# Attention followed by two feed-forward layers on one core: probabilities turned two tiles behind their scores, with four ring buffers

## What is computed

```python
scores = scale * q @ k.T + bias            # bias: relu(x @ w1 + b1) @ w2
attn = exp(scores - max); attn = attn / (sum(attn) + 1e-9)
o = attn @ v                               # 32 (batch, head) pairs of 576 x 64
h = max(x @ w1, x @ w2, x @ w3)            # x: 2304 x 512, h: 2304 x 768
x2 = h @ w_out
h2 = x2 @ w_in                             # 2304 x 2048
g = where(h2 >= 1, h2, where(h2 <= -1, 0, (h2 + 1)**2 / 4))
out = g @ w_out2
```

## Time and profile before

| | us |
|---|---|
| median of three runs | 1044.38 (1044.34 to 1044.47) |
| the profiled execution | 1044.05 |
| its span in the trace | 1042.0 |
| TensorE busy in the span | 1004.5 |
| VectorE, ScalarE, GpSimd busy | 504.7, 496.9, 293.3 |

### The profile page before, as it was taken

One profiled execution on the slowest core, in us unless ns is written; L12 is line 12 of the kernel. 1 busy time (PEld: TensorE's weight loads), 2 busy tenths in 40 slices (PEclk: granted clock), 3 DMA queues, 4 the chain that ended last, 5 costly groups with the idle time before them and its releaser, 6 DMA issues.

```text
span 1042.0 us, 20386 instructions
## 1 busy us (share of the span) xinstructions
PE 1004.5 (96%) x7608; PEld 865.7 (83%) x7608; DVE 504.7 (48%) x1172; ACT 496.9 (48%) x1024; POOL 293.3 (28%) x510
## 2 busy tenths in 40 slices
PE   6759999999998999999999999999999999999998
PEld 4447666666665999999999999998989989899997
DVE  8846666766765232313232315754454444544443
ACT  8867777877776321212121325543343443433433
POOL 1037888888874630000000234800000000000000
PEclk9978999999999999999999999999999999999999
DMA  5872432534411320000000022300000000000000
GB/s 140 260 205 65 131 83 57 151 69 127 121 25 42 122 81 1 1 0 0 0 0 0 24 73 66 122 1 31 1 31 0 0 30 0 30 0 0 31 1 31
DMA packets 96042, 56.10 MB, mean 54 GB/s; under 512 B 64224, under 2 KB 81632, under 8 KB 95968
## 3 DMA queue, kind: packets, MB, share of 16 engines
q1 hardware_dynamic: 95872, 55.11, 18.8%
q10 hardware_dynamic: 96, 0.00, 0.0%
HBM read 39.46 MB, written 15.63 MB: 53 GB/s over the span
## 4 chain that ended last, share of the span: by engine, by line
PE 89%; DMA 3%; issue 2%; ACT 2%; DVE 1%; SPq 1%; POOL 1%; ACTq 0%; DVEq 0%
PE ps L1032 41%; PE ps L1092 19%; PE ps L984 7%; PE ps L1060 7%; PE ps L932 7%; PE ps L945 4%; DMA bias_scratch<-p_t 3%; PE ps L959 1%; PE ps L908 1%; DVE s_sb L757 1%; ACT p_t L554 1%; ACT xT L545 1%; POOL probs L495 1%; PE ps L1018 1%; DMA k_in<-in_k 0%
## 5 line engine op out<-in xcount | busy, mean ns | idle before, releaser
L1032 PE MATMUL ps<-x_hi,w_all 128*128 128x384 f32 x1632 | 437.1, 336 | 1.5 <-issue 1.5
L1032 PEld LDWEIGHTS ps<-x_hi,w_all 128*128 128x128 f32 x1632 | 296.9, 188 | 6.7 <-issue 2.5
L1032 PE MATMUL ps<-x_lo,w_all 128*128 128x384 f32 x816 | 273.2, 335 | 0.0
L1092 PE MATMUL ps<-w_all,g_hi 128*128 128x512 f32 x576 | 179.7, 393 | 0.0
L514 POOL TENSOR_TENSOR w_all<-raw,w_all 128x256 fp32r<-128x256 f32 x104 | 80.2, 804 | 271.9 <-ACT w_all L637 267.2
L1032 PEld LDWEIGHTS ps<-x_lo,w_all 128*128 128x128 f32 x816 | 153.2, 188 | 3.9
L757 DVE CUSTOM_DVE_ANT_0 s_sb<-ps,bias_h 128x576 f32<-128x576 f32 (+1 forms) x160 | 114.6, 753 | 59.5 <-PE ps L932 51.2
L578 ACT ACTIVATE probs<-s_sb,row_min 128x576 f32<-128x576 f32 (+1 forms) x160 | 123.0, 769 | 5.2 <-DVE row_min L757 5.2
L1092 PEld LDWEIGHTS ps<-w_all,g_hi 128*128 128x128 f32 x576 | 106.3, 188 | 19.3 <-issue 1.2
L495 POOL TENSOR_SCALAR probs<-probs,row_inv 128x576 f32<-128x576 f32 (+1 forms) x160 | 117.8, 747 | 8.1 <-DVE row_inv L787 8.1
L1092 PE MATMUL ps<-w_all,g_lo 128*128 128x512 f32 x288 | 113.9, 396 | 0.0
(11 more groups left out here) (78 smaller groups left out, 1338.1 us busy)
## 6 DMA issues: line engine op xcount, KB each, us to landing
bias_scratch<-p_t SPq DMA_DIRECT2D x36, 296.0 KB, 3.9
raw<-in_moe_w_out SPq DMA_DIRECT2D x22, 256.0 KB, 3.1
bias_h<-bias_scratch SPq DMA_DIRECT2D x16, 288.0 KB, 4.0
raw<-in_moe_w SPq DMA_DIRECT2D x18, 256.0 KB, 3.1
out<-o_sb SPq DMA_DIRECT2D x18, 256.0 KB, 2.1
q_in<-in_q SPq DMA_DIRECT2D x32, 128.0 KB, 2.4
bias_h<-bias_scratch SPq DMA_DIRECT2D x16, 256.0 KB, 3.3
v_in<-in_v SPq DMA_DIRECT2D x32, 128.0 KB, 2.4
```

The lines of the kernel that those rows point to most:

```text
L1032: last = pe.matmul(ps[:, bank, 0:BLK], w[:, at:at + P], x[:, kt, :], start=(kt == 0 and n == 0), stop=(kt == KT - 1 and n == 2))
L1092: last = pe.matmul(ps[:, O_BANK + t, :], g[:, ft % 4, t * P:(t + 1) * P], w[:, wout_d(ft):wout_d(ft) + DM], start=(opens and i == 0), stop ...
```

## The change

LAG goes from 3 to 2 and the ring from 5 to 4. Within a slot, TensorE now runs `turn_probs` ahead of `turn_rest`, and ScalarE runs `copy_upper`, `copy_turned` and then both exponents. The `VALUES` table spreads 8, 12, 8, 8 and 4 matmuls over a group's slots, in place of 8, 8, 4, 12 and 8. q and k of group 2 are loaded ahead of the last bias loads and of v. The first block of x and the first two weight units are split in slots 71 to 79, and the first two `first_item` stand in slots 80 and 81. GpSimd's slot keeps its order.

```diff
--- before.py
+++ after.py
@@ -44,7 +44,7 @@
     PAIRS = B * H
     GROUPS = PAIRS // 2
     NU = GROUPS * NT
-    LAG = 3
+    LAG = 2
     RING = LAG + 2
     KT = DM // P
     BLK = 384
@@ -196,6 +196,7 @@
 
         SLOTS = range(NU + LAG)
         TURN = 10
+        X_SPLIT, W_SPLIT = NU - 9, NU - 5
         HALVES = (slice(0, HALF), slice(HALF, P))
 
         def ring(s):
@@ -378,6 +379,7 @@
                 if s > 4 and (s - 4) % 8 == 0:
                     first_bias(1, (s - 4) // 8 - 1, s - 4)
             first_bias(1, T - 1, NSUP - 4)
+            load_qk(2)
             for h in range(2):
                 first_bias(h, T, NSUP)
             sp.wait_ge(staged_zero, 1)
@@ -409,7 +411,7 @@
                 sp.dma_start(dst, b).then_inc(raw_in[e], 16)
 
             for i in range(GROUPS):
-                if i + 2 < GROUPS:
+                if 1 <= i < GROUPS - 2:
                     load_qk(i + 2)
                 if i:
                     load_v(i)
@@ -518,9 +520,6 @@
             for w in range(NU + 1):
                 slot(w)
 
-            pool.wait_ge(w_ok, 1)
-            low_weights(1)
-            pool.wait_ge(o_ok, PAIRS)
             pool.wait_ge(w_ok, 3)
             for u in range(3, U1 + U2):
                 low_weights(u)
@@ -612,12 +611,11 @@
                 last.then_inc(t_cp, 1)
 
             def slot(w):
+                if tile_of(w) is not None:
+                    copy_upper(tile_of(w))
                 copy_turned(w)
                 if w < NU:
                     exponent(w, 0)
-                if tile_of(w) is not None:
-                    copy_upper(tile_of(w))
-                if w < NU:
                     exponent(w, 1)
 
             def split_x(b, used, product, per_block, hi_ok):
@@ -627,7 +625,11 @@
                         act.wait_ge(used, (KT - 1) * (b - 1) + kt + 1)
                     elif used is not None:
                         act.wait_ge(product, per_block * b)
-                    act.activation(x_hi[:, kt, :], xT[:, kt, ds(b * BLK, BLK)], ACT.Copy).then_inc(hi_ok, 1)
+                    high_x(b, kt, hi_ok)
+
+            def high_x(b, kt, hi_ok):
+
+                act.activation(x_hi[:, kt, :], xT[:, kt, ds(b * BLK, BLK)], ACT.Copy).then_inc(hi_ok, 1)
 
             def split_weights(u):
                 at = unit_at(u)
@@ -645,11 +647,12 @@
                 bias_copy(s)
             for w in SLOTS:
                 slot(w)
-                if w == NU - 1:
-                    split_x(0, None, None, 0, c_x_hi)
-                if w == NU:
-                    split_weights(0)
-            split_weights(1)
+                if w == X_SPLIT:
+                    act.wait_ge(o_ok, 2 * (GROUPS - B) + 2)
+                if X_SPLIT <= w < X_SPLIT + KT:
+                    high_x(0, w - X_SPLIT, c_x_hi)
+                if w in (W_SPLIT, W_SPLIT + 2):
+                    split_weights((w - W_SPLIT) // 2)
             act.wait_ge(o_ok, PAIRS)
 
             split_weights(2)
@@ -788,7 +791,7 @@
 
             def slot(w):
                 i, t = w // NT, w % NT
-                if t == 3 and i >= 1:
+                if t == 2 and i >= 1:
                     output(i - 1, 0)
                 if t == 0 and i >= 2:
                     output(i - 2, 1)
@@ -804,9 +807,13 @@
 
             def split_x(b, hi_ok, x_ok):
                 for kt in range(KT):
-                    dve.wait_ge(hi_ok, KT * b + kt + 1)
-                    dve.tensor_tensor(x_lo[:, kt, :], xT[:, kt, ds(b * BLK, BLK)],
-                                      x_hi[:, kt, :].bitcast(F32), ALU.subtract).then_inc(x_ok, 1)
+                    low_x(b, kt, hi_ok, x_ok)
+
+            def low_x(b, kt, hi_ok, x_ok):
+
+                dve.wait_ge(hi_ok, KT * b + kt + 1)
+                dve.tensor_tensor(x_lo[:, kt, :], xT[:, kt, ds(b * BLK, BLK)],
+                                  x_hi[:, kt, :].bitcast(F32), ALU.subtract).then_inc(x_ok, 1)
 
             def low_weights(u):
 
@@ -827,8 +834,10 @@
                     first_turn()
             for w in SLOTS:
                 slot(w)
-            split_x(0, c_x_hi, c_x_ok)
-            low_weights(0)
+                if X_SPLIT + 2 <= w < X_SPLIT + 2 + KT:
+                    low_x(0, w - X_SPLIT - 2, c_x_hi, c_x_ok)
+                if w in (W_SPLIT + 2, W_SPLIT + 4):
+                    low_weights((w - W_SPLIT - 2) // 2)
             output(GROUPS - 1, 0)
             output(GROUPS - 1, 1)
             low_weights(2)
@@ -965,7 +974,7 @@
                     last = turn_in(T_BANK, at + P, k_in, j // NT % 2, j % NT)
                 last.then_inc(t_ps, 1)
 
-            VALUES = {0: (0, (0, 1)), 1: (0, (2, 3)), 2: (0, (4,)), 3: (1, (0, 1, 2)), 4: (1, (3, 4))}
+            VALUES = {0: (0, (0, 1)), 1: (0, (2, 3, 4)), 2: (1, (0, 1)), 3: (1, (2, 3)), 4: (1, (4,))}
 
             def values(i, half, units):
 
@@ -994,9 +1003,9 @@
                     scores(w)
                 if w == 0:
                     pe.wait_ge(bias_sb, NSUP)
-                turn_rest(w)
                 if tile_of(w) is not None:
                     turn_probs(tile_of(w))
+                turn_rest(w)
                 if i >= 1:
                     values(i - 1, *VALUES[t])
 
@@ -1046,10 +1055,10 @@
 
             for w in SLOTS:
                 slot(w)
-            first_item(0)
+                if w >= NU:
+                    first_item(w - NU)
             values(GROUPS - 1, 1, range(NT))
-            first_item(1)
-            first_item(2)
+            first_item(LAG)
             pe.wait_ge(o_ok, PAIRS)
 
             def c_y(n, ft, opens, closes):
```

## The result

The change is slower: 1109.29 us (median of four runs, 1108.55 to 1110.56) against 1044.36 us before on the same chip, a ratio of 1.063 with a 95% interval of 1.061 to 1.065. The profiled execution, at 1110.56 us the longest of the four, has a span of 1108.8 us, against 1042.0.

The account below looks back on a forecast made before the run. TensorE, busy 1004.5 of 1042.0 us, was taken as the bound; 1044.05 + 67.2 (attention) - 1 (end) + 8 (clock) = 1118.3, with 0.3 for the median: forecast 1119 us, own range 1100 to 1133, 8 in 10 within 1098 to 1142.

Parts of the forecast that it names:

- the loop: Attention's plain slots: TensorE turn, ScalarE copy, GpSimd high parts and normalise, back to TensorE; 3.87 us a slot against 3.22.
- the end: Last slots and first products: one slot fewer, products inside slots 80 and 81, less idle time; about 2 us back.
- shorter 64-row tiles, all groups: Attention: the 64-row tiles' shorter turns and copies give back about 0.3 us a group.
- The once-a-group wait: In 14 t = 3 slots GpSimd's high parts wait for the next slot's scores: 5.6 us, 1.73 added to the slot.
- The start: First slots: slot 2's turn at 71.4 us, half clock adds 4, and the earlier load of q and k saves nothing.
- The clock: Attention: falls to half clock behind the long gaps, 0.6 us in each of 14 groups, +8 us; bounds 0 and 34.
- A reading of the clock rows: Kernel before: full clock kept at 35 to 40 us with as many short gaps as before the fall at 67.
- only the once-a-group wait bites: Rival, attention: plain slots stay near 3.22 us and only 14 waits cost, +28 before savings; 1063 us, chance 0.07.
- the clock keeps falling: Rival, attention: the gap behind each t = 3 slot costs 2.4 us or more; 1144, up to 1160 us, chance 0.13.
- faster: Rival, attention: the loop is shorter than TensorE's slot and the new table removes VectorE's wait; 1032 us, chance 0.03.
- does not do what it says: Rival, whole kernel: all waits on `p_norm` are met late in both kernels; 1044 us, chance 0.01.
- The signs: Attention trace: groups near 21 us, `turn_probs` idle near 70 us in all, GpSimd's longest score waits in t = 3 slots.

Follow-up runs that it names:

- the extra transposes: The change plus 17 transposes of the identity, read by nobody, in each t = 4 slot from slot 9 to 79: 1105.2 us, ratio 1.059.

## Why the prediction was right

Forecast 1119 with a range of 1098 to 1142; measured 1109.3. The mechanism is shown: taking GpSimd's order out of the loop takes away 61 us, and a distance of three all of it (with the table of before); 16 us of the 77 between the change and that run are left when the order alone is changed. The size came out within 10 us partly by luck: attention was put 7 us too high and the later clock 5 too high, and the end 4 too low. The change's own trace gives the times at which the steps of the sum can be checked:

```profile
71.50 0.80 PE L954 MATMUL ps<-ident,probs 64*128 64x64 f32 x10 [3.41 <-POOL probs L497]
...
366.61 0.71 PE L954 MATMUL ps<-ident,probs 64*128 64x64 f32 x16 [0.22 <-POOL probs L497]
...
387.00 0.66 PE L954 MATMUL ps<-ident,probs 64*128 64x64 f32 x16
```

| step | forecast | measured |
|---|---|---|
| turn of slot 2 | 71.4 | 71.50 |
| plain slot of the loop | 3.87 | 3.73 |
| t = 3 slot | 5.6 | 5.52 |
| shorter 64-row tiles, all groups | -4 | about -1 |
| half clock at the start | +4 | +3.3 |
| turn of slot 73, without the later clock | 370.4, or +67.2 | 366.61 - 303.19 = +63.4, less 3 of clock: about +60.4 |
| clock behind the start | +8 | about +3 in the groups; the extra transposes gave back 4 |
| slots 73 to 79 | +1 | 387.00 - 366.61 = 20.4 against 18.9: +1.5 |
| the end | -2 | 721.8 - 719.9 = +1.9 |
| span | +74 | +66.8 |

- **The loop** was right in each piece but two. The 0.1 put between the transposes and `turn_rest` is not there: L968 follows 0.64 us behind L954's start (228.82 to 229.46). The way from GpSimd back to TensorE takes 232.55 - 232.50 = 0.05, the lower bound, not 0.1. Over 71 slots these 0.14 us are 10 us too many. The 64-row tiles give back only 0.06 us a group, not 0.3, which is 3 us the other way. The stated bounds of the sum, 3.75 to 4.0, just miss the measured 3.73; its own pieces at their low ends add up to 3.72.
- **The once-a-group wait** was 1.79 us above a plain slot, forecast 1.73.
- **The start** was right: slot 2 is due at tile 0's normalising, and slots 2 to 9 took 32.9 us where later ones take 29.6. That the earlier load saves nothing here was argued and not tested; its 5.6 us are seen at LAG 3.
- **The clock** was sized too high for this kernel: 0.6 in each group, where seven of thirteen lost nothing and five lost 0.4 to 0.8. A fall costs the change little because the slot behind the long gap has 0.87 us of idle time, which slower matmuls use up: 3.73 us became 4.2 to 4.5. In the run that normalises first in all slots but t = 3 that slot has no idle time ahead of its next turn and went from 2.7 to between 3.6 and 4.2. By the rule of the Trainium skill, page "TensorE: Matmul & The Clock Gate", section "A second HAM failure mode: psum-queue depth-cycling", that brief and frequent idling makes the clock swing, the prediction put the term nearer 34 us. The swings are there, but they cost about 3 us in the change, 11 in that run and 13 with the turns' order of before, and the two that fell more often have less idle time in their plain slots. Why, these runs don't settle.
- **A reading of the clock rows** in the prediction is not right: the stretch from 35 to 40 us does not hold as many short gaps as that from 62 to 67. It holds most of one idle piece of 1.80 us, against two of about 1 us. So it says little against that rule.

```profile
40.21 1.21 PE L1018 MATMUL ps<-xT,w2b 128*32 128x296 f32 x24 [1.80 <-DVE xT L823]
...
64.40 0.40 PE L932 MATMUL ps<-qk_hi 64*128 64x288 f32 x2 [1.00 <-DVE row_min L757]
...
67.13 0.61 PE L932 MATMUL ps<-qk_hi 64*128 64x288 f32 x2 [1.09 <-DVE row_min L757]
```

- **The end** had the wrong sign: no gain of 2 us but a loss of 1.9. Behind the turn of slot 79 TensorE idles 3.24 us for GpSimd's slow multiplication of tile 78 and 0.68 for weight unit 2, 3.9 in all, where the kernel before idles 0.8, 0.2 and 1.5 there; that is 1.4 of the 1.9. Moving the slow multiplication's cause away let a load take its place. The rest stays open.
- **The range.** The forecast's own range of 1100 to 1133 does not come out of its bounds by adding them, which gives 1102 to 1140.
- **The rivals**: "only the once-a-group wait bites" is refuted by the plain slots of 3.73 us; "the clock keeps falling" by seven groups at full clock and 4 us of gain from the extra transposes; "faster" and "does not do what it says" by the time.
- **The signs** were there: a group of 20.4 us for "near 21", TensorE's idle time ahead of `turn_probs` 2.1 us in t = 4 slots and 59 us in all for 2.2 and "near 70", and GpSimd's longest waits for scores in the t = 3 slots.

## What to carry to other kernels

Before shortening the distance between a producer and its consumer by a slot, write down each engine's order and look for what stands ahead of the producer: here a copy of other data stood ahead of `normalise`, and it depended on the very engine that was to wait. Sum the ring of handovers (3.7 us here) and set it against the slot (3.2 us); where it is longer, moving one row in one engine's order can be worth more than a better balance of work: here 61 us. Parts of a change can have opposite signs: without the shorter distance, the rest of this one was 1.1% faster than the kernel before.

## What was not expected of the hardware

- A gap of about 2 us on TensorE was followed by some 3 us at half clock in eight of thirteen groups of one kernel, at 1.0 to 1.7 us each. Seventeen useless transposes in that gap, about 2 us of extra work a group, made that kernel 11.0 us faster (1088.4 to 1077.4).
- The granted clock of one execution was 0.95 up to 197 us wherever it was not at half, which is neither of the two levels seen elsewhere; its groups were about 0.1 us longer than those at 1.00. Its cause is open.
- VectorE and GpSimd hold each other up when VectorE subtracts with both of its inputs in SBUF. Beside 128 x 1024 float32, GpSimd's pair of multiplications took 2.96 us in place of 1.47, and with the order of arrival reversed the subtraction took 1.67 in place of 1.21. It is so for the smaller subtractions of `split_x` too, which the change moved into slots 73 to 76: beside 128 x 384 the pair took 1.70 to 2.00 us. In the kernel before, where no such subtraction stands beside them, all 160 multiplications took 0.73 to 0.76 each, also beside `add_bias`, which reads PSUM.

```profile
368.08 1.77 POOL L497 TENSOR_SCALAR probs<-probs,row_inv 128x576 f32<-128x576 f32 x2 [0.71 <-DVE row_inv L790]
...
368.48 0.74 DVE L815 TENSOR_TENSOR x_lo<-xT,x_hi 128x384 fp32r<-128x384 f32 x1
```
